# Folding the low part of the last 64 keys into the fifth key chunk: probabilities times v in nine matmuls per head instead of ten

## The reference, cut to what matters

```python
scores = (q @ k^T) / sqrt(64) + bias(row, column, head)      # q, k, v: 4 x 8 heads x 576 x 64
attn   = exp(scores - max) / (sum(exp(scores - max)) + 1e-9)
x      = attn @ v                                            # then regrouped to 2304 x 512
h      = x @ w_in;  x = (h - tanh(h)) @ w_out                # first layer, 2048 wide
out    = (silu(x @ w_gate) * (x @ w_val)) @ w_out2           # second layer, 1536 wide
```

## Time and profile before

| what | value |
|---|---|
| median of 3 timed runs | 1286.54 us (1286.43 to 1287.05) |
| the profiled execution, its own time | 1287.1 us |
| its span, first to last instruction | 1285.3 us |
| TensorE matmul busy | 1202.0 us (94%), 8400 matmuls |
| TensorE weight load busy | 1133.1 us (88%) |
| VectorE busy | 639.4 us (50%) |
| ScalarE busy | 593.3 us (46%) |
| GpSimd busy | 556.2 us (43%) |
| mean granted TensorE clock | 0.98 of full |
| DMA | 125.02 MB, mean 97 GB/s |

### The profile page before, as it was taken

One profiled execution on the slowest core, in us unless ns is written; L12 is line 12 of the kernel. 1 busy time (PEld: TensorE's weight loads), 2 busy tenths in 40 slices (PEclk: granted clock), 3 DMA queues, 4 the chain that ended last, 5 costly groups with the idle time before them and its releaser, 6 DMA issues.

```text
span 1285.3 us, 25567 instructions
## 1 busy us (share of the span) xinstructions
PE 1202.0 (94%) x8400; PEld 1133.1 (88%) x8400; DVE 639.4 (50%) x1592; ACT 593.3 (46%) x1285; POOL 556.2 (43%) x656
## 2 busy tenths in 40 slices
PE   4656689999999999999999999999999999999997
PEld 2236689999999999999999999999999999999997
DVE  8976766666666666666666653521211212112111
ACT  6876645565655655656556555521212222122211
POOL 0007757677677676776776743311111111111111
PEclk9897889999999999999999999999999999999999
DMA  6875534444344444443444434400000000000000
GB/s 179 242 233 178 159 94 126 123 130 122 111 141 123 128 123 124 127 126 108 141 124 129 125 113 166 142 25 1 25 25 27 25 23 27 1 25 1 25 1 25
DMA packets 69375, 125.02 MB, mean 97 GB/s; under 512 B 8768, under 2 KB 32320, under 8 KB 69312
## 3 DMA queue, kind: packets, MB, share of 16 engines
q1 hardware_dynamic: 69312, 124.16, 32.7%
HBM read 104.07 MB, written 20.05 MB: 97 GB/s over the span
## 4 chain that ended last, share of the span: by engine, by line
PE 48%; issue 33%; POOL 8%; DVE 7%; ACT 3%; DMA 1%; POOLq 0%; SPq 0%; DVEq 0%; ACTq 0%
PE ps_h L995 14%; PE ps_y L1012 13%; PE ps_s L950 7%; PE ps_pt L963 6%; POOL fr L513 5%; PE ps_pt L973 5%; DVE feat L733 2%; PE ps_y L973 1%; DVE wbuf L725 1%; POOL prob L479 1%; POOL fr L484 1%; DVE prob L759 1%; ACT wbuf L564 1%; DVE wbuf L774 1%; DVE wbuf L720 1%
## 5 line engine op out<-in xcount | busy, mean ns | idle before, releaser
L513 POOL TENSOR_TENSOR fr<-x_stage,fr 128x384 fp32r<-128x384 f32 x72 | 73.0, 1014 | 382.4 <-ACT fr L679 382.4
L1012 PE MATMUL ps_y<-fr,wbuf 128*128 128x288 f32 x1536 | 225.4, 295 | 1.1 <-POOL fr L484 0.4
L995 PE MATMUL ps_h<-fr,wbuf 128*128 128x288 f32 x1440 | 220.1, 296 | 0.7 <-DVE fr L801 0.7
L1012 PEld LDWEIGHTS ps_y<-fr,wbuf 128*128 128x128 f32 x1536 | 210.3, 188 | 2.9 <-POOL fr L484 2.7
L479 POOL TENSOR_SCALAR prob<-prob,rowinv 96x576 f32<-96x576 f32 x192 | 145.1, 762 | 142.1 <-DVE rowinv L769 141.4
L995 PEld LDWEIGHTS ps_h<-fr,wbuf 128*128 128x128 f32 x1440 | 201.1, 189 | 1.6 <-issue 0.9
L774 DVE TENSOR_TENSOR wbuf<-ps_pt,wbuf 128x480 fp32r<-128x480 f32 x176 | 115.8, 658 | 166.2 <-ACT wbuf L564 165.5
L564 ACT ACTIVATE wbuf<-ps_pt 128x480 fp32r<-128x480 f32 x176 | 100.7, 572 | 199.8 <-PE ps_pt L963 199.4
L1094 PE MATMUL ps_y<-wbuf,fr 128*128 128x512 f32 x648 | 162.5, 395 | 1.3 <-POOL fr L513 1.3
L556 ACT ACTIVATE prob<-prob,negmax 96x576 f32<-96x576 f32 x192 | 147.8, 770 | 5.9 <-DVE negmax L759 5.4
L484 POOL TENSOR_TENSOR fr<-g_b,fr 128x288 fp32r<-128x288 f32 x128 | 112.4, 878 | 81.3 <-ACT fr L574 81.3
(11 more groups left out here) (107 smaller groups left out, 1829.5 us busy)
## 6 DMA issues: line engine op xcount, KB each, us to landing
biasb<-bias_scratch SPq DMA_DIRECT2D x192, 216.0 KB, 3.9
k_raw<-k_t SPq DMA_DIRECT2D x63, 288.0 KB, 2.8
v_raw<-v_p SPq DMA_DIRECT2D x64, 160.0 KB, 3.4
q_raw<-q_t SPq DMA_DIRECT2D x64, 144.0 KB, 2.5
biasb<-w_chunks SPq DMA_DIRECT2D x32, 256.0 KB, 3.7
prob<-w_chunks SPq DMA_DIRECT2D x8, 768.0 KB, 4.3
bias_scratch<-x_stage SPq DMA_DIRECT2D x36, 144.0 KB, 2.6
bias_scratch<-y_stage SPq DMA_DIRECT2D x36, 144.0 KB, 2.6
```

The source lines that it names most:

```text
L513: eng.tensor_tensor(a_lo[c % 2], a_b, a_hi[c % 2].bitcast(F32), ALU.subtract).then_inc(p_alo, 1)
L995: mm = eng.matmul(hidden_bank(u, c)[:, 0:T1], w[:, cols], x[:, d, :], start=d == 0 and i == 0, stop=d == KC - 1 and i == 2)
L1012: mm = eng.matmul(ps_y[:, d, 0:T1], w[:, cols], g[c % 2], start=c == 0 and i == 0, stop=c == C1 - 1 and i == 2)
```

## The change

The low part of the last 64 keys is not a chunk of its own any more. VectorE writes it into the 64 spare partitions of the fifth chunk of `pt_hi`, which held the repeated keys: a new small subtraction of 64 partitions x 96 columns reads partitions 64 to 127 and writes partitions 0 to 63, and increments a new semaphore v_ptl. The old subtraction then covers four chunks (128x384). For the product to be right, v's last 64 rows must stand in both halves of the fifth chunk. So `load_v` becomes three DMAs (four chunks of 128 rows, and the 64 rows twice, once to each half of the partitions), and `split_v` waits for 48 instead of 16. `output` waits for v_ptl too and runs nine matmuls. ScalarE's copy, GpSimd's splits and the array on the host are unchanged.

```diff
--- before.py
+++ after.py
@@ -69,8 +69,8 @@
         k_hi = wbuf[:, tail:tail + S]
         k_lo = wbuf[:, tail + S:tail + 2 * S]
         pt_at = tail + 2 * S
-        pt_hi, pt_lo = (wbuf[:, pt_at + i * JC * T1:pt_at + (i + 1) * JC * T1].rearrange("p (c t) -> p c t", c=JC)
-                        for i in range(2))
+        pt_hi, pt_lo = (wbuf[:, pt_at + i * JC * T1:pt_at + i * JC * T1 + c * T1].rearrange("p (c t) -> p c t", c=c)
+                        for i, c in enumerate((JC, JC - 1)))
 
 
 
@@ -163,7 +163,7 @@
         v_w1hi, v_w1lo, a_w2hi, v_w2lo = sem("v_w1hi"), sem("v_w1lo"), sem("a_w2hi"), sem("v_w2lo")
         e_score, v_score, a_exp, v_den, v_inv, p_norm = (sem(x) for x in (
             "e_score", "v_score", "a_exp", "v_den", "v_inv", "p_norm"))
-        e_pt, a_pt, v_pt, e_o, a_o, v_x = (sem(x) for x in ("e_pt", "a_pt", "v_pt", "e_o", "a_o", "v_x"))
+        e_pt, a_pt, v_ptl, v_pt, e_o, a_o, v_x = (sem(x) for x in ("e_pt", "a_pt", "v_ptl", "v_pt", "e_o", "a_o", "v_x"))
         a_q, v_q, p_khi, p_klo, p_vhi, p_vlo = (sem(x) for x in ("a_q", "v_q", "p_khi", "p_klo", "p_vhi", "p_vlo"))
         v_xhi, v_xlo = sem("v_xhi"), sem("v_xlo")
         e_h, a_tanh, v_g, a_ghi, p_glo, e_y, a_y = (sem(x) for x in (
@@ -342,8 +342,10 @@
 
             def load_v(n):
                 wait(eng, p_vlo, n)
-                eng.dma_start(v_raw[:, :, :], v_p[bass.ds(n % (B * H), 1), :, :]
-                              .rearrange("o p (c d) -> (o p) c d", c=JC)).then_inc(d_v, 16)
+                src = v_p[bass.ds(n % (B * H), 1), :, :].rearrange("o p (c d) -> (o p) c d", c=JC)
+                eng.dma_start(v_raw[:, 0:JC - 1, :], src[:, 0:JC - 1, :]).then_inc(d_v, 16)
+                for half in range(2):
+                    eng.dma_start(v_raw[half * D:(half + 1) * D, JC - 1, :], src[P - D:P, JC - 1, :]).then_inc(d_v, 16)
 
             def load_bias(n, par):
                 half = n // (B * H)
@@ -464,7 +466,7 @@
                 eng.tensor_tensor(lo, raw, hi.bitcast(F32), ALU.subtract).then_inc(p_klo, 1)
 
             def split_v(n, first=False):
-                eng.wait_ge(d_v, n * 16 + 16)
+                eng.wait_ge(d_v, n * 48 + 48)
                 if not first:
                     eng.wait_ge(e_o, n)
                 hold(eng)
@@ -771,8 +773,11 @@
             def pt_low(n, t, bank):
                 wait(eng, a_pt, n * NQ + (t + 1))
                 cols = slice(t * QT, (t + 1) * QT)
-                eng.tensor_tensor(pt_lo[:, :, cols], by_chunk(bank), pt_hi[:, :, cols].bitcast(F32), ALU.subtract)\
-                   .then_inc(v_pt, 1)
+                last, keys, spare = JC - 1, slice(P - D, P), slice(0, D)
+                eng.tensor_tensor(pt_hi[spare, last, cols], by_chunk(bank)[keys, last, :],
+                                  pt_hi[keys, last, cols].bitcast(F32), ALU.subtract).then_inc(v_ptl, 1)
+                eng.tensor_tensor(pt_lo[:, 0:last, cols], by_chunk(bank)[:, 0:last, :],
+                                  pt_hi[:, 0:last, cols].bitcast(F32), ALU.subtract).then_inc(v_pt, 1)
 
             def gated(m, i, bank):
                 eng.wait_ge(a_tanh, m + 1)
@@ -966,12 +971,13 @@
 
             def output(n, bank):
                 eng.wait_ge(v_pt, n * NQ + NQ)
+                eng.wait_ge(v_ptl, n * NQ + NQ)
                 eng.wait_ge(p_vlo, n + 1)
                 wait(eng, v_x, n)
-                for i, pt in enumerate((pt_hi, pt_lo)):
-                    for c in range(JC):
-                        mm = eng.matmul(bank[:, 0:T1], vv[:, c, :, :].rearrange("p a d -> p (a d)"), pt[:, c, :],
-                                        start=i == 0 and c == 0, stop=i == 1 and c == JC - 1)
+                parts = [(c, pt_hi) for c in range(JC)] + [(c, pt_lo) for c in range(JC - 1)]
+                for c, pt in parts:
+                    mm = eng.matmul(bank[:, 0:T1], vv[:, c, :, :].rearrange("p a d -> p (a d)"), pt[:, c, :],
+                                    start=(c, pt) == parts[0], stop=(c, pt) == parts[-1])
                 mm.then_inc(e_o, 1)
 
             def hidden_pieces(u, c):
```

## The result

| | before | after |
|---|---|---|
| median | 1286.43 us (11 runs, 1285.29 to 1287.56) | 1289.74 us (11 runs, 1286.61 to 1292.16) |
| ratio | | 1.0027, 95% interval 1.0019 to 1.0035 |
| profiled execution, its span | 1285.3 us | 1284.8 us |
| VectorE busy | 639.4 us | 661.7 us |

The change makes the kernel **3.3 us slower**, where 1.5 us faster was forecast; the range ended at 1288.8. First, from the page of after, its busy times and the two new groups of VectorE.

The account below looks back on a forecast made before the run. TensorE was taken to bound the full slots (99% busy), the chain of waits the plain slots. The terms -3.4 + 1.1 + 0.3 + 0.5 = -1.5 us gave 1285.0 us against the median 1286.5, range 1280.8 to 1288.8.

Parts of the forecast that it names:

- the hold: VectorE: the small subtraction's read at partition 64 makes the large one start only 0.03 us after its end.
- x: VectorE: extra time of the two subtractions over the old one for each third, 0.19 us, bounds 0.07 and 0.29.
- the matmul worth nothing in s = 7: Slot s = 7: TensorE already idles 0.91 us there, so the gap grows by what the dropped matmul saves.
- x on the path in s = 0: Slot s = 0: TensorE's second transposes wait for pt_low, adding 0.19 us in each of 6 units, +1.1 us.
- split_k not reached: Full slots: GpSimd's split_k stays off the path, slack 0.14 us after the change; the rival that it binds had chance 0.07.
- the sum of -3.4, +1.1 and +0.3 (-2.0): Full slots: s = 1 to 6 win 3.4 us, s = 0 costs 1.1, the first and last slot cost 0.3.
- 42 x 0.08: Full slots s = 1 to 6: `output` ends 0.08 us earlier in each of 42 slots, -3.4 us.
- a slack of 0.30: Full slots: scores of the second third have 0.30 us to spare after score 0, so this wait adds nothing.
- The price of a hundredth of x: Whole kernel: every 0.01 us of x is worth about 0.6 us; the sum is zero at x = 0.215.
- the step on the plain slots: Eight plain outputs: pair costs 0.29 us, matmul wins 0.22; net +0.07 each, +0.5 us, between -0.3 and +1.3.
- Not held: Rival on VectorE: the two subtractions overlap, x = 0.07, total -5.7 us, 1280.8 us; chance 0.18.
- Slower: Rival on VectorE: the small subtraction costs more than its columns, x = 0.29, +4.7 us, 1291.2 us; chance 0.13.

Follow-up runs that it names:

- second trace of after: The changed kernel run again, unchanged, for a second trace because the first was of its fastest execution: 1289.91 us.
- run 1: Kernel before with the tenth matmul of `output` left out, VectorE still doing its one subtraction: 1279.55 us, ratio 0.9943.
- run 2: Kernel before with v loaded by three DMAs as in the change, nothing else changed: 1287.47 us, ratio 1.0008.
- run 4: Changed kernel with the small subtraction reading partitions 0 to 63 in the full slots only, the plain slots keeping the shifted read: 1284.24 us, ratio 0.9987.
- run 3: Changed kernel with the small subtraction reading partitions 0 to 63 instead of 64 to 127 in all slots: 1280.01 us, ratio 0.9955.
- before, both remedies: Kernel before with `output` after all 12 hidden-layer matmuls in full slots and waiting in steps in plain slots: 1282.49 us, ratio 0.9964.

## Why the prediction was wrong, and where it was right

**Right, with its number.** The small one 0.26; the hold, and that the read causes it; x = 0.20 for 0.19; the release of `output` 0.04 for 0.05; nine matmuls 1.28 for 1.26; the matmul worth nothing in s = 7; x on the path in s = 0 (0.18 in the rows above, and the slot from s = 7's `output` to the next goes from 11.63 to 11.83); split_k not reached.

**Mis-sized, full slots: the sum of -3.4, +1.1 and +0.3 (-2.0) is +0.2 to +0.4.** Two steps failed. From `output` to `output` the two traces of after give, against before:

| place | forecast | measured, us |
|---|---|---|
| s = 1 to 6 | 42 x -0.08 = -3.4 | 41 x -0.04 = -1.6 and -1.8 |
| s = 7 to s = 0, 6 times | +1.1 | +1.15 and +1.1 |
| first and last full slot | +0.3 | +0.3 and +0.3 |
| s = 0 to s = 1, 6 times | nothing | +0.5 and +0.6 |

The term "42 x 0.08" is the first step. The slot repeats every 10.47 us, not 10.43, from 10.515. The slot won is 0.04, half of the forecast: x is a hundredth more, the nine matmuls behind the wait are two hundredths more (1.28 for 1.26), and the slot gained another hundredth less than these rows, on a difference of two nearly equal numbers. The second step is a wait at which the forecast put nothing: in the slot after a unit's end VectorE is late by x once more, and TensorE's scores of the second third wait for it. In after they start 0.05 after the end of the accumulator read in front of them; in before they start 0.16 after it, with no wait:

```profile
440.20 0.08 DVE L761 DVE_READ_ACCUMULATOR2_ANT negmax<- 96x1 f32 x1
...
440.33 0.77 PE L955 MATMUL ps_s<-wbuf,fr 128*96 128x288 f32 x4
```

The forecast had read a slack of 0.30 for this wait in another slot and used it for all. That makes the interval 10.82 for 10.72. The price of a hundredth of x, 0.6 us, had been given; the forecast took no warning from it.

**Wrong: the step on the plain slots.** It said: "one pt_low that is always on the chain (the last) and one that is in about half of the slots (the first ...): 1.5 x 0.19 = 0.29. Net +0.07, +0.5 us". By the medians it is about +4, and the chain between the plain outputs grew by 2.8/7 = 0.40 us a slot where 0.29 was forecast. Chain of waits of the second trace of after, over one plain slot from `output` to `output`:

```profile
134.47 2.54 PE ps_y L979 x9
137.03 0.41 ACT x_part L582
...
138.10 0.75 DVE prob L761
138.89 0.26 DVE wbuf L777
139.18 0.56 DVE wbuf L779
...
140.08 0.12 DVE prob L761
...
141.75 0.46 ACT wbuf L566
142.24 0.26 DVE wbuf L777
142.53 0.57 DVE wbuf L779
143.14 1.48 PE ps_y L979 x9
```

`output`, o_part and x_out, score, **pair**, score, exp, pt_high, **pair**, `output`. Of the seven stretches between plain outputs in this trace, six have two pairs on the chain and one has one, and where the first stands behind a score it is held as well. The chain of before, which I had not read slot by slot:

```profile
124.08 2.47 PE ps_y L973 x10
...
128.37 0.66 DVE wbuf L774
...
131.52 0.67 DVE wbuf L774
132.23 1.60 PE ps_y L973 x10
...
136.28 1.41 POOL fr L464
...
139.80 2.22 PE ps_y L973 x10
...
143.84 0.66 DVE wbuf L774
...
146.99 0.66 DVE wbuf L774
```

Two pt_lows from `output` to `output` there too, in six stretches of seven; only in the one after 132.23 does split_k set the end. That TensorE waits for split_k at six of its scores in this window had made me count half of the slots as covered; the chain shows that the cover is one slot. Thirteen pairs at 0.20 and three holds of 0.11 behind a score make 2.9, near the measured 2.8.

The sum for the plain slots, then. Between the first output and the eighth: the pair +2.8 where 7 x 0.29 = +2.0 was forecast, the matmul -1.2 to -1.5 as forecast (7 x -0.22 = -1.5), together +1.3 to +1.6 where +0.5 was forecast. This part is shown. By the medians of the runs, the +4 is: the matmul -1.2 (the 6.6 of run 1 less the 4.7 of (b) and 0.7 of (c)), the DMAs +1.0 (run 2; forecast 0), and the pair the rest, about +4.2; the hold alone is worth as much there by run 4. But each of these differences of medians is good to about 1 us, and they do not agree well: the kernel without the hold has the DMAs and the pair, and is only 0.5 us above that of run 1, which has neither (1.5 by the two ratios). What remains, some 2.5 us, falls to the stretches before the first output and behind the eighth, for which the forecast had no term of its own. There the chain of after passes the pair as well (once before the first output in the first trace, twice in the second, where before passes no pt_low), but the first load of k and the clock move these stretches by as much, and no run takes the three apart.

**The rivals.** "Not held" is run 3: 1280.0 us for 1280.8. "Slower" (1291.2) was right in its sign and not in its mechanism: the small instruction cost its columns and no more, and x was 0.20 in the full slots; only behind a score, where the small one is held too, does the pair come to 0.31. One of the last sentences was "The whole is wrong if a plain slot changes by more than 0.3 us, which would mean that a DMA of v or k is late there". By the medians the plain slots changed by 0.5 each, but from output to output by only 0.2, and that by VectorE. The range had taken +1.3 as the worst of the plain slots from the same 1.5.

**Open.** (c) is 0.5 to 0.9 us shorter in all traces but those of the kernel with ten matmuls and one subtraction; the second layer is the same code in all of them. Most of the difference lies at a single place, some 216 us behind the last `output`, in the second layer. There the traces of before, of "v by three DMAs" and of "before, both remedies" each have one wait of TensorE, of 0.4 to 0.5 us, that no other trace has, for nothing that the profile shows:

```profile
PE ps_s L1083 <- issue: 0.5, 1, 0.5
```

What makes it is not known. Nor is what makes an execution of the changed kernel a long one. Over the 17 executions on record (1286.6 to 1292.2 us) the longer ones are those with the lower mean granted clock (0.984 in the shortest, 0.973 in the longest; correlation -0.8), but nothing tells whether the clock is the cause or goes along with longer gaps.

## What to carry to other kernels

An instruction split in two costs its fixed part again (0.16 us here). If one half reads from other partitions than its neighbours, it costs once more, as it is held behind the instruction in front, and the one behind is held behind it: look at both neighbours, also at an accumulator read. A stage where no engine is full is priced by its chain, slot by slot, with the chain read twice: once as it is, once with the suspect made longer, since a cover in one slot is none in the others. A slack read in one slot holds for slots of the same kind only. When a wait decides, see how many hundredths its slack is, and whether moving the waiting work by a few matmuls (3.3 us here) or splitting its wait in steps (5.2 us) isn't worth more than the work saved.

## What the runs showed of the hardware

- **The order in which waits are written costs 9 us here** (1299.12 against 1289.74). With v_pt, the last to come, written first, `output` starts 0.04 after the subtraction; with it written behind two others, 0.23 after it. In the trace of the second kernel the waits for v_pt and v_ptl are two instructions of 0.05 us in front of the weight load; in that of the first there is none for them.
- **A held instruction costs at both sides.** 0.13 between the two subtractions (0.30 against 0.17 from start to start) and 0.11 behind an accumulator read.
- **In plain slots the clock alternates.** Nine matmuls take 1.46 us in one slot and 2.53 in the next, at 2.4 and 1.2 GHz (granted 1.00 and 0.50 in these windows of the second trace of after), and before does much the same with ten in 1.59 and 2.4; four extra matmuls a slot raised the mean granted clock from 0.84 to 0.94, for about 1.1 us.
